# Sparse attention and a rational MLP on one core: fewer, wider transposes, residue-ordered strided V, local X through DRAM, paced casts

## The chip, the cores and the metric

The kernel runs on one core of a Trainium2 chip. The metric is the device time of one execution in microseconds. Five engines work side by side and wait for each other through semaphores: TensorE (PE; its weight loads are listed apart as PEld), VectorE (DVE), ScalarE (ACT), GpSimd (POOL) and SyncE (SP). SP and POOL issue the DMAs; 16 DMA engines carry them out.

## The reference

Attention first, then an MLP on its result. q, k and v have the shape (8 batches, 8 heads, 576 positions, 64).

```python
scores = q @ k.transpose(0, 1, 3, 2) / sqrt(64)
rel = pos[:, None] - pos[None, :]
mask_local   = (rel >= 0) & (rel < 32)                        # heads 0 to 3
mask_strided = (rel >= 0) & (pos[None] % 32 == pos[:, None] % 32)  # heads 4 to 7
attn = softmax(where(mask, scores, -1e9))
x = (attn @ v).transpose(0, 2, 1, 3).reshape(4608, 512)
h = x @ w_in                                                  # 512 -> 2048
P = a0 + a1*h + a2*h**2 + a3*h**3
Q = 1 + |b0|*|h| + |b1|*h**2
out = (P / (Q + 1e-6)) @ w_out                                # 2048 -> 512
```

## The kernel before

All arithmetic on TensorE is in bf16. The inputs are float32 in DRAM, so `casts(b)` has POOL issue casting DMAs from DRAM to DRAM: for the local heads two heads side by side in rows of 128 (`lq`, `lk`: two DMAs each per batch), and in bulk for v and for the strided q and k. `loads(b)` then has SP load a batch into SBUF: four transposes for local q and k (`lqT`, `lkT`), six loads of V windows for the local heads (`vL`, L433), eight transposes for strided q and k (`sqT`, `skT`, one per head; two neighbouring positions lie in one row, so that even and odd positions land in the two halves of the partitions), and 32 small DMAs for strided V (`vS`, L455). Each of those takes, for all four heads, the 18 positions of one residue modulo 32 and puts them on every third partition. POOL then copies strided q into blocks of three residues (`sqP`, L445).

`attention(b)` works through six units: four local heads and two pairs of strided heads. A unit is: a mask matmul and the score matmuls into PSUM (`ps_s`), the row maximum on DVE, its subtraction as a matmul, the exponential on ACT into `pL` or `pS`, a DMA transpose of the probabilities issued by SP (`ptL` L509, `ptS` L564), the product with V into `ps_acc`, and on DVE a reciprocal and a multiplication into `xL` or `xS`. V carries a column of ones, so the product also gives the row sum. Strided X goes from `xS` to DRAM in six POOL stores (`xs`, L592).

`gather(b, xl)` fills `xt`, which holds X transposed for a chunk of 512 tokens: local X by transposes from SBUF in pieces of up to 96 rows (L615, 57 in all), strided X by two transposes per batch from DRAM (L623). There are nine chunks. `mlp1` multiplies a chunk with `Win` in 16 blocks of 128 columns, four matmuls each (L641), ACT copies each block out (L645), and per group of eight blocks nine DVE instructions (L656 to L670) and two on ACT (a logarithm and an exponential in place of the division) work out the rational function. `mlp2` multiplies with `Wout` (L683), ACT copies (L688) and POOL stores the output (L694).

The order on each engine is not the order of the program. Each operation is recorded with an estimated duration, a key and, for a DMA, an estimated transfer time (`P.op`). `schedule` is a planner: it takes for each engine, in estimated time, the ready operation with the smallest key, and so writes down a fixed order per engine. For casts the key is `b * 576 - 1500`, for loads `b * 576 - 700` and a little more, for attention `b * 576` and 96 more per unit, for the MLP of chunk c `c * 512 + 1150` and more. In the planner all DMAs share one queue (`dmafree`), and SP's issues are put at 0.15 us each. Every engine then works its list strictly in order and waits where an operand is late.

Operations depend on each other by tiles. A ring is a number of buffers used in turn; a new use of one waits for the readers of the old. `ps_s` has two buffers, `ps_acc` one, `ptL` and `ptS` two each.

Of the kernel before, what the change touches and what calls it, by code (L numbers as in the profile page):

```python
# [60 lines left out]
class Prog:  # L61
# [34 lines left out]
    def schedule(self):  # L96
# [9 lines left out]
        dmafree = 0.0  # L106
# [131 lines left out]
def bass_strided_sparse_attn__then__act_rational_pade_kernel(nc, q, k, v, moe_w_in, moe_w_out, moe_a, moe_b, out):  # L238
# [57 lines left out]
    R_lqT = ring("lqT", 4, [128, S])  # L296
    R_lkT = ring("lkT", 4, [128, S])
    SW = S // 2 + 16
    R_sqT = ring("sqT", 2, [128, HL, SW])
    R_skT = ring("skT", 2, [128, HL, SW])  # L300
    R_sqP = ring("sqP", 2, [128, HL, NBK, SB])
    R_vL = ring("vL", 2, [128, NTL, HL, 66])
    R_vS = ring("vS", 2, [128, 3, 2, HL, 2, 65])
# [74 lines left out]
    for t in R_sqT.tiles + R_skT.tiles:  # L378
        fill(t, t.t[:, :, S // 2:SW], 0.0, -9e5)


    def casts(b):
        key = b * 576 - 1500 if b else -1e5
        T_lqk[b].new()
        T_sqk[b].new()
        T_v[b].new()

        def local(pair):
            for s_t, d_t in ((q, lq), (k, lk)):
                P.op("pool", lambda e, s_t=s_t, d_t=d_t: e.dma_start(  # L390
                    d_t[b, pair, :, :].rearrange("s (hh d) -> s hh d", hh=2),
                    s_t[b, 2 * pair:2 * pair + 2, :, :].rearrange("hh s d -> s hh d")),
                    4.0, key, w=[T_lqk[b]], dma=2.4)

        def bulk(s_t, d_t, h0, t):
            n = (H - h0) * S * D
            c = 1024
            P.op("pool", lambda e: e.dma_start(
                bass.AP(tensor=d_t, offset=b * n, ap=[[c, n // c], [1, c]]),
                bass.AP(tensor=s_t.tensor, offset=s_t.offset + (b * H + h0) * S * D, ap=[[c, n // c], [1, c]])),  # L400
                1.2, key, w=[t], dma=0.9 * (H - h0) / 4)
        local(0)
        local(1)
        bulk(v, vs, 0, T_v[b])
        bulk(q, sq, HL, T_sqk[b])
        bulk(k, sk, HL, T_sqk[b])

    def weights():
# [5 lines left out]
        for j in range(4):  # L414
            P.op("pool", lambda e, j=j: e.dma_start(
                Wout[:, 4 * j:4 * j + 4, :],
                w_out[512 * j:512 * j + 512, :].rearrange("(a p) n -> p a n", p=128)),
                2.0, -4e4, w=[T_wout], dma=3.3)


    def loads(b):
        key = b * 576 - 700
        st = {}
        for pair in range(2):
            for nm, R, d_t in (("q", R_lqT, lq), ("k", R_lkT, lk)):
                t = R.next()
                st[nm, pair] = t
                P.op("sp", lambda e, t=t, d_t=d_t, pair=pair: e.dma_start_transpose(t.t[:, 0:S], d_t[b, pair, :, :]),  # L428
                     0.15, key + pair, r=[T_lqk[b]], w=[t], dma=0.85)
        vl = R_vL.next()  # L430
        for i in range(NTL):
            w0 = max(0, TQ * i - STRIDE)
            P.op("sp", lambda e, i=i, w0=w0: e.dma_start(  # L433
                vl.t[:, i, :, 0:64], vs[b, 0:HL, w0:w0 + 128, :].rearrange("h p d -> p h d")),
                0.15, key + 5, r=[T_v[b]], w=[vl], dma=0.7)
        st["vl"] = vl
        tq, tk = R_sqT.next(), R_skT.next()
        for h in range(HL):
            for t, d_t in ((tq, sq), (tk, sk)):
                P.op("sp", lambda e, t=t, d_t=d_t, h=h: e.dma_start_transpose(  # L440
                    t.t[:, h, 0:S // 2], d_t[b, h, :, :].rearrange("(c two) d -> c (two d)", two=2)),
                    0.15, key + 10, r=[T_sqk[b]], w=[t], dma=0.43)
        qp = R_sqP.next()
        for h in range(HL):
            P.op("pool", lambda e, h=h: e.tensor_copy(  # L445
                qp.t[:, h, :, :].rearrange("p b (t i) -> p b t i", i=3),
                bass.AP(tensor=tq.t, offset=h * SW, ap=[[HL * SW, 128], [3, NBK], [16, TT], [1, 3]])),
                0.7, key + 11, r=[tq], w=[qp])
        st["sq"], st["sk"] = qp, tk
        vS = R_vS.next()  # L450
        for i in range(16):
            blk, i3 = divmod(i, 3)
            base = 64 * (blk % 2) + i3
            for par in range(2):
                P.op("sp", lambda e, i=i, par=par, blk=blk, base=base: e.dma_start(  # L455
                    vS.t[base:base + 52:3, blk // 2, par, :, blk % 2, 0:64],
                    bass.AP(tensor=vs, offset=((b * H + HL) * S + 2 * i + par) * D,
                            ap=[[32 * D, TT], [S * D, HL], [1, D]])),
                    0.15, key + 12, r=[T_v[b]], w=[vS], dma=0.1)
# [3 lines left out]
    def attention(b, st):  # L463
# [4 lines left out]
        for kind, idx in (("L", 0), ("S", 0), ("L", 1), ("S", 2), ("L", 2), ("L", 3)):  # L468
# [5 lines left out]
            if kind == "L":  # L474
                h = idx
                pb_ = 64 * (h % 2)
                tq, tk = st["q", h // 2], st["k", h // 2]

                def score(e, tq=tq, tk=tk, pb_=pb_, pst=pst):
# [4 lines left out]
                    for i in range(NTL):  # L484
# [11 lines left out]
                def negm(e, ng=ng, pst=pst):  # L496
                    r = None
                    for j, n in ((0, 4), (1, 2)):
# [11 lines left out]
                     0.15, key, r=[pp], w=[pt], dma=0.83)  # L510
# [18 lines left out]
            tq, tk = st["sq"], st["sk"]  # L529

            def score(e, tq=tq, tk=tk, idx=idx, pst=pst):
# [4 lines left out]
                for j in range(2):  # L536
                    for blk in range(NBK):
                        for par in range(2):
                            kc = tk.t[64 * par:64 * par + 64, idx + j, 3 * blk:3 * blk + 288]
# [11 lines left out]
            def negm(e, ng=ng, pst=pst):  # L551
                r = None
                for j in range(2):
# [11 lines left out]
                 0.15, key, r=[pp], w=[pt], dma=1.1)  # L565
            for j in range(2):
# [37 lines left out]
    def gather(b, xl):  # L604
        key = b * 576 + 550
        for i in range(NTL):
            r0 = 0
            while r0 < TQ:
                g0 = b * S + i * TQ + r0
                c, col = divmod(g0, CH)  # L610
                n = min(TQ - r0, CH - col)
                if r0 == 32:
                    n = min(n, 32)
                t = chunk_tile(c)
# [142 lines left out]
```

How the kernel before makes its waits and increments, by code:

```python
            def go(eng):  # L200
                for ws, o in queues[e]:
                    for s, n in ws:
                        eng.wait_ge(s, n)
                    inst = o.maker(eng)
                    if o.dma is not None:
                        inst.then_inc(o.dst.sem, 16)
                    elif inst is not None:
                        inst.then_inc(sems[e], 1)
# [6 lines left out]
        def pool(eng):  # L215
            run("pool")(eng)
            for s, n in fin.items():
                eng.wait_ge(s, n)
```

## Time and profile before

| | |
|---|---|
| Median of three executions | 778.69 us (777.74 to 779.48) |
| Profiled execution | 781.19 us, span 779.0 us, 6110 instructions |
| Busy: PE, DVE, ACT, POOL | 395.9, 362.0, 267.7, 141.1 us |
| Mean granted TensorE clock | 0.861 |
| DMA issues of vS, of xt from xL, of vL | 256, 57, 48 |

Times on the page are microseconds from the first instruction of the profiled execution. Busy time is the time in which an engine had an instruction under way; issuing a DMA from SP is not counted as busy, and stands as SPq. The chain of waits is followed back from the last instruction: at each step to what released it. In a timeline, the name behind an arrow in brackets is what ended the idle time before an instruction. The granted clock is a share of 2.4 GHz, 0.5 being the lower level of 1.2 GHz.

### The profile page before, as it was taken

The numbers are of one execution on the slowest core, as the hardware profiler recorded it, in microseconds if no ns is written. First come the engines' busy times: TensorE is split into PE (matmuls) and PEld (weight loads), VectorE is DVE, ScalarE is ACT, GpSimd is POOL, SyncE is SP. The second block draws the span as 40 slices with busy tenths as digits, with TensorE's granted clock in tenths as the row PEclk, the third lists the DMA queues.
The fourth block names the chain that finished last, engine by engine and source line by source line (L and its number), as shares of the span: only waits on it lengthen the run. The fifth ranks groups of instructions, "written<-read, shape, count | busy, mean of one in ns | idle before, by whom it ended". The sixth has DMA issues, their size and how long they took to land.

```text
span 779.0 us, 6110 instructions
## 1 busy us (share of the span) xinstructions
PE 395.9 (51%) x2304; PEld 178.2 (23%) x2304; DVE 362.0 (46%) x353; ACT 267.7 (34%) x265; POOL 141.1 (18%) x184
## 2 busy tenths in 40 slices
PE   0212240401565010890169095789089959699864
PEld 0001120200222000340024042344034424233321
DVE  3000130100309104360298086489088959969960
ACT  0100000100126040262057044458138657577740
POOL 9007034005160100120003002022010400301100
PEclk9999999999997555795579588799579979999988
DMA  9999969218899042232301342352141321301011
GB/s 148 197 146 116 153 91 111 46 28 127 109 138 123 12 79 53 66 74 39 70 9 53 57 91 48 71 101 60 29 88 30 76 67 39 83 13 55 27 41 40
DMA packets 186076, 58.44 MB, mean 75 GB/s; under 512 B 179552, under 2 KB 182144, under 8 KB 185536
## 3 DMA queue, kind: packets, MB, share of 16 engines
q0 software_dynamic: 46144, 30.17, 23.3%
q1 hardware_dynamic: 139904, 27.90, 22.4%
q8 instruction: 18, 0.29, 0.2%
q14 instruction: 10, 0.08, 0.0%
HBM read 42.54 MB, written 25.95 MB: 88 GB/s over the span
## 4 chain that ended last, share of the span: by engine, by line
SPq 49%; PE 18%; DVE 17%; DMA 6%; ACT 4%; issue 4%; POOL 0%; DVEq 0%; ACTq 0%; POOLq 0%
SPq L455 24%; SPq L440 9%; PE ps_out L683 8%; PE ps_h L641 7%; SPq L615 7%; SPq L433 4%; SPq L428 4%; DVE z L666 3%; DVE z L668 3%; DMA ptL<-pL 3%; DVE h L670 2%; DVE u L660 2%; SPq L509 2%; DVE z L667 1%; ACT u L661 1%
## 5 line engine op out<-in xcount | busy, mean ns | idle before, releaser
L683 PE MATMUL ps_out<-Wout,h 128*128 128x512 bf16 x576 | 148.3, 411 | 25.6 <-ACT os L688 13.1
L641 PE MATMUL ps_h<-xt,Win 128*128 128x512 bf16 x576 | 144.2, 403 | 22.2 <-ACT h L645 9.4
L645 ACT ACTIVATE h<-ps_h 128x512 bf16<-128x512 f32 x144 | 85.0, 597 | 107.4 <-PE ps_h L641 107.3
L516 PE MATMUL ps_acc<-vL,ptL 128*96 128x65 bf16 x192 | 17.5, 237 | 165.3 <-DMA ptL<-pL 163.0
L505 ACT ACTIVATE pL<-ps_s 96x768 bf16<-96x768 f32 x32 | 25.7, 803 | 218.5 <-DMA ptL<-pL 121.4
L522 DVE RECIPROCAL rc<-ps_acc 96x6 f32<-96x6 f32 x32 | 6.1, 189 | 189.0 <-PE ps_acc L516 188.9
L694 POOL DMA_DIRECT2D out_dram<-os x36 | 26.5, 736 | 344.6 <-ACT os L688 340.2
L683 PEld LDWEIGHTS ps_out<-Wout,h 128*128 128x128 bf16 x576 | 57.0, 104 | 103.2 <-issue 17.1
L641 PEld LDWEIGHTS ps_h<-xt,Win 128*128 128x128 bf16 x576 | 52.0, 103 | 98.4 <-ACT h L645 30.4
L661 ACT ACTIVATE u<-u,consts 128x4096 bf16<-128x4096 bf16 x18 | 66.6, 3702 | 2.3 <-DVE u L660 2.2
L663 ACT ACTIVATE u<-u 128x4096 bf16<-128x4096 bf16 x18 | 65.1, 3618 | 0.1
L592 POOL DMA_DIRECT2D xs<-xS x48 | 35.4, 742 | 155.8 <-DVE xS L583 155.7
L493 DVE TENSOR_REDUCE ng<-ps_s 96x6 bf16<-96x768 f32 x32 | 30.3, 946 | 60.7 <-PE ps_s L487 60.6
L516 PEld LDWEIGHTS ps_acc<-vL,ptL 128*96 128x96 bf16 x192 | 15.6, 155 | 174.1 <-DMA ptL<-pL 166.9
L688 ACT ACTIVATE os<-ps_out 128x512 f32<-128x512 f32 x36 | 21.5, 596 | 98.6 <-PE ps_out L683 98.5
L481 PE MATMUL ps_s<-ML,IDN 128*96 128x512 bf16 x64 | 21.2, 423 | 57.4 <-DMA lkT<-lk 31.8
L445 POOL COPY sqP<-sqT 128x324 bf16<-128x324 bf16 x32 | 18.5, 620 | 128.0 <-DMA sqT<-sq 128.0
L390 POOL DMA_DIRECT2D lk<-in_k_dram x16 | 41.4, 3070 | 0.0
L524 DVE TENSOR_TENSOR xL<-ps_acc,rc 96x384 bf16<-96x384 f32 x32 | 17.6, 549 | 51.2 <-DMA xt<-xs 48.7
L660 DVE TENSOR_TENSOR u<-u,z 128x4096 bf16<-128x4096 bf16 x18 | 41.1, 2286 | 0.3
L666 DVE TENSOR_TENSOR z<-z,h 128x4096 bf16<-128x4096 bf16 x18 | 41.0, 2279 | 0.2
L670 DVE TENSOR_TENSOR h<-z,u 128x4096 bf16<-128x4096 bf16 x18 | 41.1, 2282 | 0.1
(41 smaller groups left out, 474.5 us busy)
## 6 DMA issues: line engine op xcount, KB each, us to landing
out_dram<-os POOLq DMA_DIRECT2D x36, 256.0 KB, 2.5
v<-in_v_dram POOLq DMA_DIRECT2D x8, 576.0 KB, 10.3
vS<-v SPq DMA_DIRECT2D x256, 9.0 KB
vL<-v SPq DMA_DIRECT2D x48, 64.0 KB, 2.2
lq<-in_q_dram POOLq DMA_DIRECT2D x16, 144.0 KB, 11.5
lk<-in_k_dram POOLq DMA_DIRECT2D x16, 144.0 KB, 11.3
sq<-in_q_dram POOLq DMA_DIRECT2D x8, 288.0 KB, 10.6
sk<-in_k_dram POOLq DMA_DIRECT2D x8, 288.0 KB, 11.8
```

What stands on the lines that cost most here:

```text
L390: P.op("pool", lambda e, s_t=s_t, d_t=d_t: e.dma_start(d_t[b, pair, :, :].rearrange("s (hh d) -> s hh d", hh=2), s_t[b, 2 * pair:2 * pair ...
L440: P.op("sp", lambda e, t=t, d_t=d_t, h=h: e.dma_start_transpose(t.t[:, h, 0:S // 2], d_t[b, h, :, :].rearrange("(c two) d -> c (two d)", t ...
L455: P.op("sp", lambda e, i=i, par=par, blk=blk, base=base: e.dma_start(vS.t[base:base + 52:3, blk // 2, par, :, blk % 2, 0:64], bass.AP(tens ...
L615: P.op("sp", lambda e, t=t, r0=r0, n=n, col=col, i=i: e.dma_start_transpose(t.t[:, 0:2, col:col + n], xl.t[r0:r0 + n, i, :]), 0.15, key + ...
L641: r = e.matmul(ph.t[:, :], Win[:, kk, f * 128:(f + 1) * 128], xt.t[:, kk, :], start=(kk == 0), stop=(kk == NK1 - 1))
L645: P.op("act", lambda e, f=f, ph=ph, h=h: e.activation(h.t[:, f % G, :], ph.t[:, :], AF.Copy), 0.53, key, r=[ph], w=[h])
L660: dv(lambda e, zz=zz, uu=uu: e.tensor_tensor(uu, uu, zz, op=Alu.mult), tt, r=[z], m=[u])
L661: P.op("act", lambda e, uu=uu: e.activation(uu, uu, AF.Ln, bias=eps1, scale=1.0), 0.833 * W / 1000 + 0.28, key, r=[T_co], m=[u])
L663: P.op("act", lambda e, uu=uu: e.activation(uu, uu, AF.Exp, scale=-1.0), 0.833 * W / 1000 + 0.19, key, m=[u])
L666: dv(lambda e, zz=zz, hh=hh: e.tensor_tensor(zz, zz, hh, op=Alu.mult), tt, r=[h], m=[z])
L670: dv(lambda e, zz=zz, hh=hh, uu=uu: e.tensor_tensor(hh, zz, uu, op=Alu.mult), tt, r=[z, u], m=[h])
L683: r = e.matmul(po.t[:, :], groups[g].t[:, j, m * 128:(m + 1) * 128], Wout[:, kk, :], start=(kk == 0), stop=(kk == NF - 1))
```

## The change

Local q and k of a batch stand in one DRAM tensor (`lqk16`) and come in by one transpose of 2304 rows into `lT`; strided q and k likewise, through `sqk16` into `sT`. V of the local heads is cast in bulk. V of the strided heads is cast by 13 DMAs into `vp16`, whose rows are already in the order of blocks and residues, and six DMAs load it into `vS`. Local X is stored to DRAM by one POOL DMA into the left half of each row of `xs16`, and `gather` has two transposes per batch for whole rows. The casts of batch b + 2 are recorded after attention(b) and wait for the first score of batch b. The rings of `ptL` and `ptS` have three buffers. The planner has one DMA queue per issuing engine, and new durations for SP; the key of the `Wout` loads goes from -4e4 to -300.

```diff
-        dmafree = 0.0
+        dmafree = {e: 0.0 for e in self.ENG}
...
-                dmafree = max(dmafree, t + o.dur) + o.dma
-                o.fin = dmafree + 2.2
+                dmafree[e] = max(dmafree[e], t + o.dur) + o.dma
+                o.fin = dmafree[e] + 2.2
...
-    R_ptL = ring("ptL", 2, [128, NTL, TQ])
-    R_ptS = ring("ptS", 2, [128, 2 * 3, 128])
+    R_ptL = ring("ptL", 3, [128, NTL, TQ])
+    R_ptS = ring("ptS", 3, [128, 2 * 3, 128])
...
+        pace = [first_score[b - 2]] if b - 2 in first_score else []
+
+        def po(fn, dur, t, dma):
+            o = P.op("pool", fn, dur, key, w=[t], dma=dma)
+            for d in pace:
+                o.deps[d] = 1
...
-        bulk(v, vs, 0, T_v[b])
-        bulk(q, sq, HL, T_sqk[b])
-        bulk(k, sk, HL, T_sqk[b])
+        bulk(v, vl16, b * n, 0, n, T_v[b])
+        bulk(q, sqk, b * 2 * n, HL, n, T_sqk[b])
+        bulk(k, sqk, (b * 2 + 1) * n, HL, n, T_sqk[b])
+        vo = b * NBK * SB * HL * 128
+        for h in range(HL):
+            for i3 in range(3):
+                so = v.offset + (b * H + HL + h) * S * D + i3 * 2 * D
+                po(lambda e, h=h, so=so, i3=i3: e.dma_start(
+                    bass.AP(tensor=vp16, offset=vo + (i3 * HL + h) * 128,
+                            ap=[[3 * HL * 128, TT], [SB * HL * 128, 5], [1, 128]]),
+                    bass.AP(tensor=v.tensor, offset=so, ap=[[32 * D, TT], [6 * D, 5], [1, 128]])),
+                    0.75, T_vp[b], 0.25)
+        po(lambda e: e.dma_start(
...
-        for pair in range(2):
-            for nm, R, d_t in (("q", R_lqT, lq), ("k", R_lkT, lk)):
...
-                P.op("sp", lambda e, t=t, d_t=d_t, pair=pair: e.dma_start_transpose(t.t[:, 0:S], d_t[b, pair, :, :]),
-                     0.15, key + pair, r=[T_lqk[b]], w=[t], dma=0.85)
+        lt = R_lT.next()
+        P.op("sp", lambda e: e.dma_start_transpose(
+            lt.t[:, :, :, :].rearrange("p a b s -> p (a b s)"), lqk[b, :, :, :, :].rearrange("a b s d -> (a b s) d")),
+            1.4, key, r=[T_lqk[b]], w=[lt], dma=3.4)
...
-        for h in range(HL):
-            for t, d_t in ((tq, sq), (tk, sk)):
-                P.op("sp", lambda e, t=t, d_t=d_t, h=h: e.dma_start_transpose(
+        P.op("sp", lambda e: e.dma_start_transpose(
+            sT.t[:, 0:2 * HL * SW], bass.AP(tensor=sqk, offset=b * 2 * HL * S * D, ap=[[128, 2 * HL * SW], [1, 128]])),
+            1.4, key + 10, r=[T_sqk[b]], w=[sT], dma=3.4)
...
-        for i in range(16):
-            blk, i3 = divmod(i, 3)
-            base = 64 * (blk % 2) + i3
-            for par in range(2):
+        for blk in range(NBK):
+            base = 64 * (blk % 2)
+            n = SB if blk < 5 else TT
+            hi = base + SB if blk < 5 else base + 52
+            P.op("sp", lambda e, blk=blk, base=base, n=n, hi=hi: e.dma_start(
+                vS.t[base:hi:(1 if n == SB else 3), blk // 2, :, :, blk % 2, 0:64],
+                vp16[b, blk, 0:n, :].rearrange("p (h two d) -> p h two d", h=HL, two=2)),
+                0.7, key + 12, r=[T_vp[b]], w=[vS], dma=0.4)
...
+        P.op("pool", lambda e: e.dma_start(
+            bass.AP(tensor=xs, offset=b * S * Fin, ap=[[Fin, TQ], [TQ * Fin, NTL], [1, 256]]), xl.t[0:TQ, :, :]),
+            1.5, base + 500, r=[xl], w=[T_xs[b]], dma=1.5)
...
-                P.op("sp", lambda e, t=t, r0=r0, n=n, col=col, i=i: e.dma_start_transpose(
-                    t.t[:, 0:2, col:col + n], xl.t[r0:r0 + n, i, :]), 0.15, key + i, r=[xl], w=[t], dma=0.3)
...
-                t.t[:, 2:4, col:col + n], xs[b, r0:r0 + n, :]), 0.15, key + 10, r=[T_xs[b]], w=[t], dma=1.5 * n / 512)
+                t.t[:, :, col:col + n], xs[b, r0:r0 + n, :]), 1.3, key + 10, r=[T_xs[b]], w=[t], dma=3.0 * n / 512)
...
     weights()
-    for b in range(1, B):
-        casts(b)
+    casts(1)
...
+        if b + 2 < B:
+            casts(b + 2)
```

## Rows read from the trace of the kernel before

**Rows 1.** The page: busy time with share and instructions; the chain's shares.
```profile
PE 395.9 (51%) x2304; PEld 178.2 (23%) x2304; DVE 362.0 (46%) x353; ACT 267.7 (34%) x265; POOL 141.1 (18%) x184
...
SPq 49%; PE 18%; DVE 17%; DMA 6%; ACT 4%; issue 4%; POOL 0%; DVEq 0%; ACTq 0%; POOLq 0%
SPq L455 24%; SPq L440 9%; PE ps_out L683 8%; PE ps_h L641 7%; SPq L615 7%; SPq L433 4%; SPq L428 4%; DVE z L666 3%; DVE z L668 3%; DMA ptL<-pL 3%; DVE h L670 2%; DVE u L660 2%; SPq L509 2%; DVE z L667 1%; ACT u L661 1%
```

**Rows 2.** SP's timeline, 143 to 300 us: start, duration of the group, line, operation, count.
```profile
143.79 25.06 SPq L455 DMA_DIRECT2D vS<-v  x32
...
180.46 3.33 SPq L433 DMA_DIRECT2D vL<-v  x6
...
218.88 2.59 SPq L623 DMA_TRANSPOSE xt<-xs  x2
...
290.85 8.91 SPq L615 DMA_TRANSPOSE xt<-xL  x7
```

**Rows 3.** Views by tile, lqT and sqT: issue in ns, least/median/most; first and last start.
```profile
L428 SPq DMA_TRANSPOSE lqT<-lq x16: 1146/1263/11241, 11.2 to 527.9; - x16
...
L440 SPq DMA_TRANSPOSE sqT<-sq x32: 1149/1245/5744, 47.4 to 335.0; - x32
```

**Rows 4.** SP's timeline at the start, 28 to 86 us.
```profile
28.94 12.61 SPq L433 DMA_DIRECT2D vL<-v  x6
...
80.11 5.92 SPq L509 DMA_TRANSPOSE ptL<-pL  x2
```

**Rows 5.** TensorE's timeline: first and third mask matmul, first product, first MLP, late MLP.
```profile
31.80 0.87 PE L481 MATMUL ps_s<-ML,IDN 128*96 128x512 bf16 x2 [31.80 <-DMA lkT<-lk]
...
42.06 0.88 PE L481 MATMUL ps_s<-ML,IDN 128*96 128x512 bf16 x2 [0.90 <-ACT pL L505]
...
89.94 0.69 PE L516 MATMUL ps_acc<-vL,ptL 128*96 128x65 bf16 x6 [20.52 <-DMA ptL<-pL]
...
224.43 15.48 PE L641 MATMUL ps_h<-xt,Win 128*128 128x512 bf16 x64
...
514.68 3.62 PE L683 MATMUL ps_out<-Wout,h 128*128 128x512 bf16 x16
```

**Rows 6.** Windows: length, busy time of PE, PEld, DVE, ACT, POOL; clock, DMA share, GB/s.
```profile
0.00:230.00 230.00, 58.08 (x397) 28.18 (x398) 34.24 (x63) 15.83 (x21) 75.53 (x96) 1.00 0.85 117
230.00:300.00 70.00, 18.13 (x102) 7.50 (x100) 22.84 (x17) 22.93 (x19) 4.77 (x4) 0.63 0.62 71
460.00:700.00 240.00, 180.37 (x1067) 81.75 (x1066) 177.87 (x165) 137.08 (x136) 36.09 (x45) 0.87 0.27 59
690.00:752.00 62.00, 50.49 (x223) 20.26 (x220) 60.91 (x36) 46.42 (x41) 5.98 (x8) 0.97 0.09 34
752.00:779.00 27.00, 14.20 (x56) 5.42 (x56) 0.73 (x1) 2.39 (x4) 2.16 (x4) 0.84 0.10 39
```

**Rows 7.** POOL's timeline: copies of strided q, starts of three casts, stores of strided X.
```profile
60.07 1.78 POOL L445 COPY sqP<-sqT 128x324 bf16<-128x324 bf16 x4 [39.58 <-DMA sqT<-sq]
...
64.12 3.06 POOL L390 DMA_DIRECT2D lk<-in_k_dram  x1
64.91 2.79 POOL L398 DMA_DIRECT2D v<-in_v_dram  x1
65.40 2.79 POOL L398 DMA_DIRECT2D sq<-in_q_dram  x1
...
334.32 3.93 POOL L592 DMA_DIRECT2D xs<-xS  x6 [5.31 <-DVE xS L583]
```

**Rows 8.** DMA view: all packets; issues of strided transposes, count and median us to landing.
```profile
DMA packets 186076, 58.44 MB, mean 75 GB/s; under 512 B 179552, under 2 KB 182144, under 8 KB 185536
...
sqT<-sq SPq DMA_TRANSPOSE x32, 2.5
```

**Rows 9.** Groups of instructions by line: shapes, count, busy us, mean ns, idle time before.
```profile
L683 PE MATMUL ps_out<-Wout,h 128*128 128x512 bf16 x576 | 148.3, 411 | 25.6 <-ACT os L688 13.1
L641 PE MATMUL ps_h<-xt,Win 128*128 128x512 bf16 x576 | 144.2, 403 | 22.2 <-ACT h L645 9.4
```

More of the change, by code:

```diff
@@ L280, in bass_strided_sparse_attn__then__act_rational_pade_kernel @@
     T_v = [Tile(f"v{b}") for b in range(B)]
+    T_vp = [Tile(f"vp{b}") for b in range(B)]
     T_xs = [Tile(f"xs{b}") for b in range(B)]
@@ L295, in bass_strided_sparse_attn__then__act_rational_pade_kernel @@
     T_b = Tile("babs")
[L296 to L300, printed above, removed]
+    R_lT = ring("lT", 2, [128, 2, 2, S])
+    SW = S // 2
+    R_sT = ring("sT", 2, [128, 2 * HL * SW + 16])
     R_sqP = ring("sqP", 2, [128, HL, NBK, SB])
     R_vL = ring("vL", 2, [128, NTL, HL, 66])
-    R_vS = ring("vS", 2, [128, 3, 2, HL, 2, 65])
+    R_vS = ring("vS", 2, [128, 3, HL, 2, 2, 65])
     R_pL = ring("pL", 3, [128, NTL * 128])
     R_pS = ring("pS", 2, [128, 2 * NBK * 64])
-    R_ptL = ring("ptL", 2, [128, NTL, TQ])
-    R_ptS = ring("ptS", 2, [128, 2 * 3, 128])
+    R_ptL = ring("ptL", 3, [128, NTL, TQ])
+    R_ptS = ring("ptS", 3, [128, 2 * 3, 128])
     R_xL = ring("xL", 2, [128, NTL, HL * D])
@@ L377, in bass_strided_sparse_attn__then__act_rational_pade_kernel @@
         fill(t, t.t[:, :], 0.0, -9e5)
-    for t in R_sqT.tiles + R_skT.tiles:
-        fill(t, t.t[:, :, S // 2:SW], 0.0, -9e5)
+    for t in R_sT.tiles:
+        fill(t, t.t[:, 2 * HL * SW:], 0.0, -9e5)
+    first_score = {}
     def casts(b):
@@ L386, in casts @@
         T_v[b].new()
[L388 to L401, printed above, removed]
@@ L402, in casts, with bulk @@
-        local(0)
-        local(1)
-        bulk(v, vs, 0, T_v[b])
-        bulk(q, sq, HL, T_sqk[b])
-        bulk(k, sk, HL, T_sqk[b])
+        T_vp[b].new()
+        pace = [first_score[b - 2]] if b - 2 in first_score else []
[3 more added lines that the diff above has]
+                o.deps[d] = 1
+        def bulk(s_t, d_t, off, h0, n, t):
+            c = n // 128
+            po(lambda e: e.dma_start(
+                bass.AP(tensor=d_t, offset=off, ap=[[c, 128], [1, c]]),
+                bass.AP(tensor=s_t.tensor, offset=s_t.offset + (b * H + h0) * S * D, ap=[[c, 128], [1, c]])),
+                1.0, t, 1.9)
@@ new lines, in casts @@
+        n = HL * S * D
+        for pair in range(2):
+            for qk, s_t in ((0, q), (1, k)):
+                po(lambda e, s_t=s_t, qk=qk, pair=pair: e.dma_start(
+                    lqk[b, qk, pair, :, :].rearrange("s (hh d) -> s hh d", hh=2),
+                    s_t[b, 2 * pair:2 * pair + 2, :, :].rearrange("hh s d -> s hh d")), 3.1, T_lqk[b], 2.4)
+        bulk(v, vl16, b * n, 0, n, T_v[b])
+        bulk(q, sqk, b * 2 * n, HL, n, T_sqk[b])
+        bulk(k, sqk, (b * 2 + 1) * n, HL, n, T_sqk[b])
@@ L476, in attention, with score @@
                 pb_ = 64 * (h % 2)
-                tq, tk = st["q", h // 2], st["k", h // 2]
-                def score(e, tq=tq, tk=tk, pb_=pb_, pst=pst):
+                lt = st["lt"]
+                pr = h // 2
+                def score(e, lt=lt, pr=pr, pb_=pb_, pst=pst):
                     for j, n in ((0, 4), (1, 2)):
@@ L528, in attention @@
                 continue
-            tq, tk = st["sq"], st["sk"]
+            tq, tk = st["sq"], st["sT"]
             def score(e, tq=tq, tk=tk, idx=idx, pst=pst):
@@ L602, in chunk_tile, with gather @@
         return xt_of[c]
-    def gather(b, xl):
+    def gather(b):
         key = b * 576 + 550
[L606 to L614, printed above, removed]
-                P.op("sp", lambda e, t=t, r0=r0, n=n, col=col, i=i: e.dma_start_transpose(
-                    t.t[:, 0:2, col:col + n], xl.t[r0:r0 + n, i, :]), 0.15, key + i, r=[xl], w=[t], dma=0.3)
-                r0 += n
         r0 = 0
@@ L707, in bass_strided_sparse_attn__then__act_rational_pade_kernel @@
             st = loads(b + 1)
-        xl = attention(b, cur)
-        gather(b, xl)
+        attention(b, cur)
+        gather(b)
+        if b + 2 < B:
+            casts(b + 2)
         while nxt < NCH and (nxt + 1) * CH <= (b + 1) * S:
```

60 lines of the change are left out of this document (29 added, 31 removed).

## The prediction

> **What bounds the kernel now.** I read the chain of waits first. Its summary [rows 1] gives 49% of the span to SPq, the time that SP's sequencer needs to issue DMAs; matmuls and VectorE have 18% and 17%. The largest single line is L455, the strided-V pieces, with 24%. So no engine's arithmetic is the bound over the whole run: VectorE is busy for 46% and TensorE for 51% [rows 1].
>
> The timeline of SP [rows 2] says what an issue costs, and the views by tile [rows 3] give its spread. A transpose takes 1.24 to 1.29 us (8.91 / 7 = 1.27 for `xt<-xL`, 2.59 / 2 for `xt<-xs`), a piece of vL 3.33 / 6 = 0.56, a piece of vS 25.06 / 32 = 0.78. The medians are the same for 288 rows (sqT, 1245 ns) and 576 rows (lqT, 1263 ns). One batch therefore occupies SP for: lqT and lkT 4 x 1.27 = 5.1; vL 3.3; sqT and skT 8 x 1.25 = 10.0; vS 25.1; six probability transposes 7.5; 57 / 8 = 7.1 transposes of local X 9.1; two of strided X 2.6. The sum is 62.7 us, eight batches 502 us of the span of 779.0.
>
> Two places show what that does. At the start [rows 4, 5] the first score runs at 31.80, but SP is then busy with vL (12.61 us), with the strided transposes and with vS, so the first probability transpose is issued at 80.11, the first probabilities meet V at 89.94, and the first matmul of the MLP comes at 224.43. In the windows [rows 6] VectorE works 34.24 of the first 230 us, 178 of 240 in the middle (74%), and 60.91 of 62 (98%) in the stretch of MLP alone near the end. That last stretch holds two chunks of the MLP, 31 us each; behind it 27 us are left in which VectorE is done.
>
> **The change, part by part.**
>
> SP. Twelve transposes of q and k become two: 15.1 us becomes 2 x c. The shape, four times the largest here, is not in the trace. Below, c is an issue's 1.25; above, it grows with the rows and is 4 x 1.27 = 5.1. Since a doubling from 288 to 576 rows adds 0.02 us [rows 3], I take 1.4. The 32 vS pieces become 6: each between vL's 0.56 and 54 / 18 of 0.78 = 2.3 us; they move as many runs as a vL piece, so I take 0.7, together 4.2. The 7.1 transposes of xL go, and the two that stay are twice as wide, 1.3 each (at most 2.6). vL (3.3) and the six probability transposes (7.5) stay. The new sum is 2.8 + 4.2 + 3.3 + 7.5 + 2.6 = 20.4 us per batch, 163 us in all, against 502 before. SP stops being the bound. With all upper ends it is 10.2 + 13.8 + 3.3 + 7.5 + 5.2 = 40 us, still under what VectorE needs per batch (below).
>
> POOL. Starts of successive casts lie 0.79 us apart for the local ones (64.12 to 64.91) and 0.49 for the bulk ones; a store of strided X costs 3.93 / 6 = 0.66 [rows 7]. Added per batch are 13 casts of strided V in 72 or 90 short rows, each between 0.49 and 0.79 (I take 0.6: 7.8 us), and one store of local X (0.7). That is 8.5 us per batch on an engine busy for 18% [rows 1]; the cover is its idle time. What stands queued behind: a cast paced by the first score of two batches earlier holds up the sqP copies and stores behind it. Before, casts stood behind the copies the same way, POOL waiting 39.58 us once [rows 7]; bound 0 to 40 us once at the start, 0 taken, because score(0) is early.
>
> DMA. The bytes stay but for local X, 2.4 MB more written, on 58.44 MB [rows 8]. Pacing moves casts of batches 2 to 7 out of the first 230 us, when the engines had a share of 0.85, to where the share was 0.27 [rows 6]. The probability transposes there get slower neighbours; I put that into the utilisation below.
>
> Planner. SP's real durations now stand in its costs, so each queue's order should fit better; DMA is split into two independent queues, which fits worse. I cannot price either from a row: between 0 and the difference of 74% and 98%.
>
> **The start.** The four local casts still come first, so the first score stays at 31.8 (a transpose that lands as a whole could make it 5 us later; weights behind more casts, 5 earlier). vL ends at 41.6 as before, the strided transpose adds 2, and the first probability transpose goes at about 45 instead of 80.1. First use at 45 + 9.8 (80.11 to 89.94) = 55. Strided: sqP was copied at 60.07 [rows 7], behind eight transposes; behind one it comes about eight issues less one earlier, at 60 - 8.8 = 51, and at 56 if the wide one lands late, which I take. Scores follow each other at half of 42.06 - 31.80 [rows 5], two take 10.3; then again 9.8: X is whole at 76. Seven stores (4.6) and a landing (2.5, as sqT's [rows 8]) make 83, two transposes and a landing 88: there the first MLP matmul stands, not at 224. Eight blocks of four matmuls at up to twice 0.226 us [rows 5] later, and a little for the copies, VectorE starts on the MLP at about 105, or 97 if the level is high; I take 97, as its first group is fed while attention of batch 1 keeps TensorE busy. Ends: 75 if DMA clears sooner, 140 if stores wait on POOL.
>
> **What is late next.** VectorE has 362.0 us of work [rows 1]. At 97 it has done the fills and about two batches of attention; the 34.24 us before 230 contained about three, so I subtract 27 and leave 335. TensorE is as loaded: MLP matmuls at the high level take 3.62 / 16 = 0.226 us [rows 5], times 1152 = 260 us; attention has 395.9 - 148.3 - 144.2 = 103 us [rows 1, 9], six eighths of it 78: together 338. Two engines of equal load that feed each other, with transposes between, won't reach the 98% of the MLP stretch; with SP gone they should beat the 74%. I take the middle, 86%: 335 / 0.86 = 390. Sum: 97 + 390 + 27 = 514 us of span. The profiled execution was 781.19 us (2.2 more than its span) and the median is 778.69, so 514 + 2.2 - 2.5 = **514 us** as a median. Ends of the likeliest case: with the early start and 93%, 75 + 335 / 0.93 + 27 = 462 (98% was seen only without attention beside it); 97 + 335 / 0.74 + 27 = 577 above.
>
> The page "DMA: Bandwidth & Descriptors" of the Trainium skill (section "Issuing engines are not separate DMA queues") says that DMAs from several engines interleave on the same 16 DMA engines, and that the issue time saved is usually small beside the transfer. By its second half SP's relief would buy little; the SP rows here speak against that, since 502 us of issue lie mostly on the chain. Its first half speaks against the planner's split queues and for the first rival.
>
> **The rivals.**
>
> 1. The DMA engines become the bound. 60.8 MB must move. With shares scaled to one, the start carried 117 / 0.85 = 138 GB/s and the stretch from 230 to 300 carried 71 / 0.62 = 115 [rows 6]. Then 60.8 MB takes 440 to 529 us, and one chunk (31) and the tail (27) follow the last X, some output stores lying beside: about 500 to 587, 565 at the poor mix. For it: casts now run beside everything. Against it: a share of 0.27 in the middle. Chance 0.18.
>
> 2. TensorE stays at the low level. Between 230 and 300 the granted clock was 0.63 with TensorE busy 18 of 70 us; it was 0.97 in 690 to 752 with 50 of 62 [rows 6]. From 1.2 GHz a matmul takes about twice its 0.226. At a mean granted clock of 0.75, 338 / 0.75 = 451 us; at 90% use 501, plus 97 + 27 = 625; with the VectorE bound still partly beside it, 580 to 640. Against it: fewer long waits. Chance 0.10.
>
> The page "TensorE: Matmul & The Clock Gate" of the Trainium skill (section "Part 1: The HAM clock gate") says that the throttled clock is the default and that activity releases it; by that rule, a denser kernel loses this rival, and the two windows agree with it.
>
> 3. SP stays the bound, because the wide transposes are issued as slowly as their rows: 40 us per batch, and at the start, vL's pieces took 12.61 / 6 = 2.1 us under the cast flood [rows 4]; with that all along, 10 more, 50 per batch. 8 x 50 + 97 + 31 + 27 = 555. Against: medians flat in the rows [rows 3], and 5.1 per four transposes already counts it. Chance 0.06.
>
> 4. Slower: the pacing turns the prefetch into a chain. If POOL holds the casts of batch b+2 behind stores that wait for the end of batch b or b+1, each batch runs cast, landing, transpose, score, attention one behind the other. From cast to first score it took 31.8 us at the start [rows 5], and attention with its issues took at most the 62.7 us of SP: 94.5 per batch, 8 x 94.5 + 31 + 27 = 814. It decides from (778.7 - 58) / 8 = 90 us per batch. For it: POOL issues in order, with 22 more issues between. Against: casts have two batches' lead and 47 us per batch of cover. Chance 0.03.
>
> **How the numbers follow.** The forecast (462 to 577) has 0.62, rival 1 (500 to 590) 0.18, rival 2 (580 to 640) 0.10, rival 3 (about 555) 0.06, rival 4 0.03, and 0.01 for no change. The range runs from 462, where about 0.08 lies below, to 595, where most of rival 2 and all of rival 4 lie above (0.12). About 0.2% is what can be told from no change here: faster 0.96, same 0.01, slower 0.03.
>
> **What would show it.** Right: SPq drops from 49% of the chain to under 15%, with vS in 6 issues of 0.6 to 0.9 us per batch; both wide transposes at 1.3 to 1.6 us; the first MLP matmul between 75 and 110; VectorE at 80 to 92% from there to the tail; DMA share about 0.6 to 0.8, spread evenly. Wrong: first MLP matmul after 140; VectorE waiting on xt or on probability transposes for over 80 us; POOL idle on a pace wait while SP waits for casts; a granted clock under 0.8 from 100 us on; wide transposes of 5 us.

## The result and the profile after

The changed kernel takes 574.52 us in the median of its runs (567.13 to 586.55), against 778.22 before; the ratio is 0.7325, with a 95% interval of 0.7258 to 0.7391. The profiled execution took 567.13 us, with a span of 565.2. Two of its four executions (576.16 and 586.55 us) were slow ones and the ratio is formed without them, so it lies a little under 574.52 / 778.22. The forecast of 514 was 60 us too low, and the range 462 to 595 holds the time.

The page of the changed kernel, to set beside [rows 1]: busy times, then the chain by engine and by line.

```profile
PE 377.1 (67%) x2268; PEld 175.1 (31%) x2304; DVE 363.6 (64%) x351; ACT 265.5 (47%) x265; POOL 235.2 (42%) x296
...
PE 31%; DVE 20%; SPq 16%; ACT 14%; DMA 14%; issue 3%; POOL 1%; POOLq 0%
PE ps_h L648 13%; PE ps_out L690 10%; ACT u L670 5%; SPq L448 5%; ACT u L668 5%; SPq L453 5%; DMA ptS<-pS 4%; DMA ptL<-pL 4%; DMA lT<-lqk 3%; DVE u L667 3%; SPq L468 3%; DVE z L673 2%; ACT h L652 2%; DVE z L675 2%; DVE h L677 2%
```

SPq fell from 49% to 16% of a chain that is 214 us shorter. Its place is taken by TensorE, VectorE and, new at this size, DMA with 14%.

SP's timeline shows the issues of a quiet batch, from 340 us on, and four of the crowded start (as [rows 2, 4]).

```profile
30.68 14.04 SPq L453 DMA_TRANSPOSE sT<-sqk  x1
...
54.36 3.99 SPq L524 DMA_TRANSPOSE ptL<-pL  x3
...
149.01 2.07 SPq L441 DMA_TRANSPOSE lT<-lqk  x1
...
169.78 5.51 SPq L630 DMA_TRANSPOSE xt<-xs  x2
...
340.02 2.43 SPq L453 DMA_TRANSPOSE sT<-sqk  x1
...
343.97 2.04 SPq L441 DMA_TRANSPOSE lT<-lqk  x1
...
358.33 4.70 SPq L468 DMA_DIRECT2D vS<-vp  x6
...
366.49 3.35 SPq L448 DMA_DIRECT2D vL<-vl  x6
...
376.00 3.65 SPq L630 DMA_TRANSPOSE xt<-xs  x2
```

In a quiet batch SP needs 2.4 + 2.0 + 4.7 + 3.4 + 3.7, and six probability transposes at their median of some 1.25, so 23.7 us, where 20.4 was forecast. The views by tile (as [rows 3]: least, median, most, in ns) have the spread: a wide transpose costs 2.0 us at its cheapest and 14 in the crowd, a vS piece 0.74 whether it has 18 or 54 partitions.

```profile
L441 SPq DMA_TRANSPOSE lT<-lqk x8: 2038/4382/13748, 11.0 to 344.0; - x8
...
L453 SPq DMA_TRANSPOSE sT<-sqk x8: 2088/2774/14045, 30.7 to 340.0; - x8
...
L468 SPq DMA_DIRECT2D vS<-vp x48: 739/740/3234, 44.8 to 362.3; - x48
```

The windows (as [rows 6]) cut the run where the forecast cut it: until the first MLP matmul, until VectorE's first MLP instruction, until its last, and the tail.

```profile
0.00:180.00 180.00, 63.87 (x451) 33.40 (x453) 42.33 (x78) 16.83 (x21) 106.67 (x159) 1.00 1.29 147
180.00:197.00 17.00, 12.32 (x41) 4.69 (x39) 0.76 (x3) 5.36 (x9) 6.01 (x11) 0.80 0.98 149
197.00:540.00 343.00, 287.54 (x1725) 131.76 (x1759) 320.49 (x271) 240.92 (x231) 120.32 (x126) 0.96 0.49 90
540.00:565.20 25.20, 13.39 (x54) 5.20 (x53) 0.00 (x0) 2.39 (x4) 2.16 (x4) 0.84 0.11 42
```

After 197 us VectorE is busy for 320.49 of 343 us, 93%, at a granted clock of 0.96: this part is better than forecast. Before it, VectorE has 43 us of work in 197, while the DMA engines have a share of 1.29 until 180 us (the times of packets overlap, since the share passes 1). The start was forecast at 97 us. TensorE's timeline of the start (as [rows 5]) has the steps of that forecast, and POOL's timeline the stores of X.

```profile
21.07 0.88 PE L494 MATMUL ps_s<-ML,IDN 128*96 128x512 bf16 x2 [21.07 <-DMA lT<-lqk]
...
57.02 0.69 PE L531 MATMUL ps_acc<-vL,ptL 128*96 128x65 bf16 x6 [22.07 <-DMA ptL<-pL]
72.54 0.84 PE L494 MATMUL ps_s<-ML,IDN 128*96 128x512 bf16 x2 [14.84 <-DMA lT<-lqk]
...
75.90 0.85 PE L549 MATMUL ps_s<-MS,IDN 128*128 128x384 bf16 x2
...
179.78 3.19 PE L648 MATMUL ps_h<-xt,Win 128*128 128x512 bf16 x7 [1.01 <-DMA xt<-xs]
```

```profile
123.73 1.78 POOL L458 COPY sqP<-sT 128x324 bf16<-128x324 bf16 x4 [16.65 <-DMA sT<-sqk]
125.44 0.79 POOL L604 DMA_DIRECT2D xs<-xL  x1
126.21 3.68 POOL L611 DMA_DIRECT2D xs<-xS  x6
```

The first score came at 21 us (forecast 31.8) and the first product at 57 (55). Then it parts: the strided scores of batch 0 stand in TensorE's order behind a score of batch 1, whose lT lands at 72.5. The stores of X stand on POOL behind the copies for batch 2, which wait 16.65 us for its sT, and the transposes into xt are issued at 169.78, on SP behind the loads of batch 3. The first MLP matmul is at 179.78, not 88. Some 40 us of that lie between the last store of X(0), issued by 130, and its transposes at 169.78: in that time SP works off its list, the loads of batch 3 from 149.01 on among it.

### The profile page after: what moved, and what is told of

The parts are those of the page before. It is cut to its first block, busy times and chain, and to the rows that moved or that the text cites. A ratio compares the mean times of both kernels' runs of the same rounds, so it can differ in the third digit from the quotient of the medians.

```text
span 565.2 us, 5814 instructions
## 1 busy us (share of the span) xinstructions
PE 377.1 (67%) x2268; PEld 175.1 (31%) x2304; DVE 363.6 (64%) x351; ACT 265.5 (47%) x265; POOL 235.2 (42%) x296
## 4 chain that ended last, share of the span: by engine, by line
PE 31%; DVE 20%; SPq 16%; ACT 14%; DMA 14%; issue 3%; POOL 1%; POOLq 0%
PE ps_h L648 13%; PE ps_out L690 10%; ACT u L670 5%; SPq L448 5%; ACT u L668 5%; SPq L453 5%; DMA ptS<-pS 4%; DMA ptL<-pL 4%; DMA lT<-lqk 3%; DVE u L667 3%; SPq L468 3%; DVE z L673 2%; ACT h L652 2%; DVE z L675 2%; DVE h L677 2%
## 5 line engine op out<-in xcount | busy, mean ns | idle before, releaser
L648 PE MATMUL ps_h<-xt,Win 128*128 128x512 bf16 x560 | 141.6, 401 | 26.5 <-ACT h L652 18.7
L690 PE MATMUL ps_out<-Wout,h 128*128 128x512 bf16 x556 | 132.5, 385 | 28.1 <-ACT os L695 13.5
L701 POOL DMA_DIRECT2D out_dram<-os x36 | 34.8, 1177 | 159.0 <-ACT os L695 155.0
L414 POOL DMA_DIRECT2D vp<-in_v_dram x96 | 88.2, 3558 | 0.0
L690 PEld LDWEIGHTS ps_out<-Wout,h 128*128 128x128 bf16 x576 | 54.2, 99 | 94.6 <-ACT os L695 16.9
L458 POOL COPY sqP<-sT 128x324 bf16<-128x324 bf16 x32 | 30.1, 1532 | 89.5 <-DMA sT<-sqk 89.5
L611 POOL DMA_DIRECT2D xs<-xS x48 | 43.8, 1060 | 53.4 <-DVE xS L599 53.4
L675 DVE TENSOR_TENSOR z<-z,h 128x4096 bf16<-128x4096 bf16 x18 | 41.3, 2294 | 0.2
L667 DVE TENSOR_TENSOR u<-u,z 128x4096 bf16<-128x4096 bf16 x18 | 41.1, 2286 | 0.2
L404 POOL DMA_DIRECT2D lqk<-in_k_dram x16 | 41.3, 2923 | 0.0
L673 DVE TENSOR_TENSOR z<-z,h 128x4096 bf16<-128x4096 bf16 x18 | 41.0, 2277 | 0.2
L663 DVE TENSOR_SCALAR z<-h 128x4096 uint16<-128x4096 uint16 x18 | 21.9, 1217 | 24.1 <-ACT h L652 24.1
```

The source lines that it names most:

```text
L404: po(lambda e, s_t=s_t, qk=qk, pair=pair: e.dma_start(lqk[b, qk, pair, :, :].rearrange("s (hh d) -> s hh d", hh=2), s_t[b, 2 * pair:2 * pa ...
L414: po(lambda e, h=h, so=so, i3=i3: e.dma_start(bass.AP(tensor=vp16, offset=vo + (i3 * HL + h) * 128, ap=[[3 * HL * 128, TT], [SB * HL * 128 ...
L611: P.op("pool", lambda e, p0=p0, nb=nb, i3=i3, par=par: e.dma_start(bass.AP(tensor=xs, offset=(b * S + 2 * i3 + par) * Fin + 256, ap=[[32 * ...
L648: r = e.matmul(ph.t[:, :], Win[:, kk, f * 128:(f + 1) * 128], xt.t[:, kk, :], start=(kk == 0), stop=(kk == NK1 - 1))
L667: dv(lambda e, zz=zz, uu=uu: e.tensor_tensor(uu, uu, zz, op=Alu.mult), tt, r=[z], m=[u])
L673: dv(lambda e, zz=zz, hh=hh: e.tensor_tensor(zz, zz, hh, op=Alu.mult), tt, r=[h], m=[z])
```

## The experiments

All ratios are to the kernel before; the changed kernel's is 0.7325 (0.7258 to 0.7391). Two theories for the late start: the planner's order, since its costs for POOL's issues are up to four times the measured ones; or the DMA engines, full with casts and loads of batches that are not needed yet.

**e1_cost.** POOL's costs in the planner as measured.

```diff
-                    ... 3.1, T_lqk[b], 2.4)
+                    ... 0.79, T_lqk[b], 2.4)
...
-                    0.75, T_vp[b], 0.25)
+                    0.62, T_vp[b], 0.25)
...
```

> The changed kernel with POOL's measured issue times in the planner (local cast 0.79 instead of 3.1 us, bulk 0.5 instead of 1.0, strided V 0.62 instead of 0.75, stores 0.79 and 0.63 instead of 1.5 and 0.75). Theory order: VectorE is idle before 180 us because the planner overprices POOL and so puts strided scores, stores of X and xt late; first MLP matmul at about 140 instead of 180, time 530 to 550. Theory flood: the DMA engines are full until 180 us whatever the order; first MLP matmul at 170 or later, time 560 to 580.

Measured: ratio 0.7229 (0.7166 to 0.7291), median 561.35 us. The interval meets that of the changed kernel, so a gain of up to some 2% isn't shown. The first MLP matmul came at 174.28, and VectorE's first MLP instruction at 184.15 instead of 197, with 342 us from there to the end of its last in both. So the costs hold at most 13 of the 100 us by which the start is late.

**e2_two.** No casts for batches 2 to 7.

```diff
     def loads(b):
         key = b * 576 - 700
+        b = b % 2
...
-        if b + 2 < B:
-            casts(b + 2)
```

> The changed kernel with the casts of batches 2 to 7 left out; their loads read the casts of batch 0 or 1, so X is wrong for six batches and all other work is the same. Theory flood: casts fill the DMA engines for the first 180 us; without them the first MLP matmul comes at 110 to 130 and the time is 490 to 520. Theory order: the order is nearly the same, so the first MLP matmul stays at 150 or later and the time at 540 or more.

Measured: 0.6468 (0.6435 to 0.6502), 502.4 us; the first MLP matmul at 120.60. Windows of this run, cut at the same events:

```profile
0.00:120.00 120.00, 48.62 (x368) 25.74 (x368) 31.98 (x58) 13.49 (x17) 47.81 (x77) 1.00 1.10 150
120.00:132.00 12.00, 12.00 (x70) 5.49 (x69) 4.92 (x9) 5.97 (x10) 3.63 (x6) 1.00 0.69 134
132.00:473.00 341.00, 299.97 (x1818) 135.57 (x1817) 323.40 (x285) 243.72 (x234) 79.14 (x90) 0.96 0.39 86
473.00:498.00 25.00, 12.71 (x53) 4.91 (x51) 0.00 (x0) 2.39 (x4) 2.16 (x4) 0.84 0.11 42
```

The middle and the tail are as long as in the changed kernel (341 and 25 us, against 343 and 25); the whole difference of 67 us of span lies before VectorE's first MLP instruction (130.06 against 196.99; the window is cut 2 us behind it). Up to the first MLP matmul the engines moved 120 x 150 = 18.0 MB here and 180 x 147 = 26.5 MB there, at about one rate. So the casts of later batches are what makes the first X late by these 67 us.

How they do it is not settled by this run, for the order did not stay nearly the same, as I had expected it to. SP's timeline of this run:

```profile
111.92 3.35 SPq L631 DMA_TRANSPOSE xt<-xs  x2
115.32 2.66 SPq L442 DMA_TRANSPOSE lT<-lqk  x1
```

Here the transposes of X(0) stand ahead of the lT and the vS of batch 3; in the changed kernel (149.01, then 169.78) they stand behind all its loads, which wait for its casts. Fewer bytes and an earlier place on SP came together; e11_novp, below, comes nearest to parting them.

**e3_nopace.** The wait for the first score is left out.

```diff
-        pace = [first_score[b - 2]] if b - 2 in first_score else []
+        pace = []
```

> The changed kernel without the wait of casts(b) for the first score of batch b-2. If the pacing spreads the casts: the casts go out earlier, DMA share over 1 in the first 150 us, first MLP matmul later than 190, time 580 to 610. If POOL's order alone paces them already (copies of strided q stand between two batches of casts): same within 1%, 560 to 580.

Measured: 0.7381 (0.7353 to 0.7409), no difference shown. That wait paces nothing: in POOL's timeline of this run, as in the changed kernel's, the copies, which wait for sT, already stand between two batches of casts.

**e8_pacex.** Measured costs, and a later pace: the casts of batch b+2 wait for the last multiplication of attention(b).

```diff
-        pace = [first_score[b - 2]] if b - 2 in first_score else []
+        pace = [last_x[b - 2]] if b - 2 in last_x else []
...
```

> The changed kernel with POOL's measured issue times in the planner (as e1_cost) and the casts of batch b+2 waiting for the last multiplication of attention(b) instead of its first score. Theory flood: with only two batches of casts in the way, the first MLP matmul comes at 115 to 135, as in e2_two, and the later casts are hidden: 510 to 530. Rival: the prefetch becomes too short, TensorE waits on lT or vS in every batch after 200 us: 555 or more.

Measured: 0.7648 (0.7603 to 0.7694), slower. The first MLP matmul came at 141.22, but VectorE then worked 87.47 and 81.34 of 120 us in two windows, and POOL waited for the pace, four times and 41.1 us in all. The profiled run, at 603.19 us, is the longest of four and 1.7% over the shortest, which is far less than what lies between 70% and the 93% of the changed kernel.

```profile
180.00:300.00 120.00, 84.44 (x509) 37.72 (x508) 87.47 (x86) 61.88 (x56) 67.54 (x77) 0.84 0.81 118
300.00:420.00 120.00, 84.71 (x532) 39.78 (x530) 81.34 (x80) 58.57 (x58) 55.53 (x71) 0.86 0.84 116
```

```profile
POOL lqk L405 <- DVE xL L540: 41.1, 4, 18.8
```

**e10_pace2.** Measured costs, and the later pace for batches 2 and 3 alone: they wait for the end of attention(0).

```diff
-        pace = [first_score[b - 2]] if b - 2 in first_score else []
+        pace = [last_x[0]] if b in (2, 3) else [first_score[b - 2]] if b > 3 else []
...
```

> As e1_cost, with the casts of batches 2 and 3 alone waiting for the end of attention(0). Theory flood with prefetch kept later: first MLP matmul at 135 to 145 as in e8_pacex, VectorE over 90% busy after 180 as in e1_cost: 525 to 545. Rival: batch 2 then comes late and the time is lost between 180 and 300: 560 or more.

Measured: 0.7514 (0.7458 to 0.757), slower. The first MLP matmul came at 179.98, no earlier than without: casts of two batches then went out together, with a DMA share of 1.42 from 120 to 180. The bytes were moved, not removed: 27.2 MB by the first MLP matmul.

**e11_novp.** No strided V casts for batches 2 to 7.

```diff
+        if b > 1:
+            return
         vo = b * NBK * SB * HL * 128
...
```

> The changed kernel with the 13 casts of strided V left out for batches 2 to 7 (their vS loads read batch 0 or 1, so the strided heads of six batches are wrong). If the new small casts cost by their bytes, a sixth of the casts: 10 to 14 us less, 555 to 565. If short pieces cost much more than their bytes: 30 us less or more, 545 or below.

Measured: 0.7269 (0.721 to 0.7328); not told apart from the changed kernel, with the first MLP matmul at 152.04. The new small casts alone are not what costs the 67 us of e2_two, but they have a part in the start: VectorE's first MLP instruction came at 163 against 197, though X(0)'s transposes still stood behind the lT and the sT of batch 3.

This run also shows that an early first matmul is not yet a short run. From VectorE's first MLP instruction to its last it took 377 us against 342, with the same work. The first loss is chunk 1:

```profile
185.86 3.60 PE L650 MATMUL ps_h<-xt,Win 128*128 128x512 bf16 x8 [14.02 <-DMA xt<-xs]
```

The granted clock over these 377 us was 0.90, against 0.96. Only in e2_two, where casts are gone from the whole run, did the time behind the start stay as short.

**e4_oldvs.** Strided V as before, the rest changed.

```diff
-        for blk in range(NBK):
+        for i in range(16):
+            blk, i3 = divmod(i, 3)
...
+            for par in range(2):
+                P.op("sp", ... 0.78, key + 12, r=[T_v[b]], w=[vS], dma=0.1)
...
```

> The changed kernel with strided V as before: one bulk cast of all V and 32 loads per batch of 0.78 us on SP, with that duration in the planner; the 13 casts per batch on POOL go. SP gets 20 us more per batch (about 41 in all). If SP's occupancy is the bound as long as it nears the 47 us per batch of VectorE: 600 to 650. If SP at 41 us stays hidden and the 13 casts cost as much in the DMA engines: 555 to 585.

Measured: 0.787 (0.783 to 0.7909), 617.27 us. SP's timeline of this run and TensorE's, then waits of PEld: the first row is this run's, the other two are the changed kernel's (us in all, times, longest):

```profile
80.21 26.40 SPq L454 DMA_DIRECT2D vS<-vl  x32
106.66 1.27 SPq L511 DMA_TRANSPOSE ptL<-pL  x1
...
137.16 24.03 SPq L454 DMA_DIRECT2D vS<-vl  x28
161.23 3.33 SPq L617 DMA_TRANSPOSE xt<-xs  x2
```

```profile
109.32 0.69 PE L518 MATMUL ps_acc<-vL,ptL 128*96 128x65 bf16 x6 [28.88 <-DMA ptL<-pL]
...
165.92 3.59 PE L635 MATMUL ps_h<-xt,Win 128*128 128x512 bf16 x8 [25.00 <-DMA xt<-xs]
```

```profile
PEld ps_h L635 <- DMA xt<-xs: 46.9, 5, 25.6
...
PEld ps_acc L531 <- DMA ptL<-pL: 35.7, 6, 22.7
PEld ps_h L648 <- DMA xt<-xs: 7.0, 2, 6.2
```

Two blocks of vS stand on SP ahead of something that TensorE waits for: 26.40 us ahead of a probability transpose, 24.03 ahead of the transposes into xt. The waits for local probabilities did not grow: this run has the one of 28.88 us, the changed kernel 35.7 in all. What grew is the wait for xt, from 7.0 to 46.9 us.

**e5_narrow**, the wide transposes cut into twelve, and **e6_oldx**, local X from SBUF with four buffers for xL.

```diff
-        P.op("sp", lambda e: e.dma_start_transpose(
-            lt.t[:, :, :, :].rearrange("p a b s -> p (a b s)"), ...
+        for pair in range(2):
+            for qk in range(2):
+                P.op("sp", lambda e, ...: e.dma_start_transpose(
+                    lt.t[:, qk, pair, :], lqk[b, qk, pair, :, :]), 1.27, ...
...
```

```diff
-                t.t[:, :, col:col + n], xs[b, r0:r0 + n, :]), 1.3, ...
+                t.t[:, 0:2, col:col + n], xl.t[r0:r0 + n, i, :]), 1.27, ...
...
+                t.t[:, 2:4, col:col + n], xs[b, r0:r0 + n, :]), 1.3, ...
```

> The changed kernel with the two wide transposes per batch cut into twelve as before (4 of 576 rows, 8 of 288), at 1.27 and 1.25 us in the planner. SP gets about 10 us more per batch. If SP has slack now: 560 to 585, as the changed kernel. If SP's occupancy still counts: 600 to 630. The wide transposes took 2.0 to 4.4 us to issue, not 1.4; if that is the DMA queue pushing back, the narrow ones will add up to the same per batch.

> The changed kernel with local X transposed from SBUF in 57 pieces as before (1.27 us each in the planner), and four buffers for xL. SP gets about 9 us more per batch, the DMA engines 2.4 MB less. SP has slack: 560 to 580. SP counts: 590 to 620, with VectorE or PE waiting on xt.

Measured: 0.74 (0.7349 to 0.7451) and 0.7268 (0.7236 to 0.73). Neither is told apart from the changed kernel.

**e9_joint.** Both at once.

> The changed kernel with both e5 and e6: twelve narrow transposes and 57 transposes of local X from SBUF. SP gets about 19 us more per batch, as much as the old strided V gave it in e4_oldvs. If what e4 lost is SP's occupancy as such: 605 to 625, as e4. If it is the block of 32 issues ahead of a probability transpose, 25 us at a stretch: 570 to 585, as e5 and e6 alone.

Measured: 0.7381 (0.7313 to 0.7449), 577.79 us, again not told apart. SP's timeline of this run:

```profile
94.05 2.71 SPq L584 DMA_TRANSPOSE ptS<-pS  x2
...
130.87 11.10 SPq L636 DMA_TRANSPOSE xt<-xL  x8
...
148.82 5.13 SPq L443 DMA_TRANSPOSE lT<-lqk  x4
153.99 10.97 SPq L456 DMA_TRANSPOSE sT<-sqk  x8
```

With vS (4.7), vL (3.1), two xt (2.6) and the probabilities (7.5) that is 45 us per batch, as much as in e4_oldvs, where vS takes 25 and the rest some 19. But it costs nothing that these runs can show, and e4 costs 43 us in the median. So the occupancy of SP as such has stopped to count at this size. What e4 has and e9 has not are the waits for xt (46.9 us against 1.3). That the place of the vS blocks ahead of xt costs the 43 us is read from these waits; no run kept e4's loads and moved them.

**b1_spcost.** The kernel before, with SP's measured issue times in the planner and four buffers for xL; no DMA is changed.

```diff
-                    0.15, key + 12, r=[T_v[b]], w=[vS], dma=0.1)
+                    0.78, key + 12, r=[T_v[b]], w=[vS], dma=0.1)
...
```

> The kernel before with SP's measured issue times in the planner (1.24 to 1.29 us for transposes, 0.55 for vL, 0.78 for vS instead of 0.15), and four buffers for xL; no DMA changed. If the kernel before was bound by SP's occupancy of 502 us: 740 to 780, hardly faster. If a good part was the order that the planner wrote with SP at 0.15 us: 620 to 700.

Measured: 0.9146 (0.9111 to 0.9182), 712.84 us, between the two ranges expected. Its chain still is SP's:

```profile
SPq 46%; PE 24%; DVE 17%; DMA 5%; ACT 4%; issue 3%; POOL 0%; POOLq 0%
SPq L455 22%; PE ps_h L641 13%; PE ps_out L683 7%; SPq L440 7%; SPq L615 6%; SPq L428 5%; SPq L433 4%; DVE z L668 3%; DVE z L666 3%; DVE h L670 3%; DMA xt<-xs 2%; DVE u L660 2%; DVE z L667 2%; DVE z L664 1%; DVE z L656 1%
```

So honest costs and the buffers, which were not tried apart, bring 66 of the 204 us with every DMA as before. What fell is TensorE's wait for local probabilities, while its wait for xt from xs rose, from 8.1 to 58.5 us. The first row is from the kernel before, the second from this run:

```profile
PE ps_acc L516 <- DMA ptL<-pL: 163.0, 10, 23.8
...
PE ps_acc L516 <- DMA ptL<-pL: 42.7, 4, 16.8
```

**e12_cshared.** e1_cost with one DMA queue in the planner, as before the change.

```diff
-        dmafree = {e: 0.0 for e in self.ENG}
+        dmafree = 0.0
...
```

> As e1_cost, with one DMA queue for all engines in the planner again, as before the change. If the 16 DMA engines are shared in fact, the planner's order gets better: 540 to 553. If its one queue is too strict (all transfers one after another, probability transposes behind casts): 570 to 600.

Measured: 0.7387 (0.733 to 0.7444), against 0.7229 (0.7166 to 0.7291) for e1_cost: some 12 us more, with the intervals apart. But VectorE's first MLP instruction is earlier here (178.6 against 184.2); the time is lost behind it, at a granted clock of 0.91 against 0.96, and the two kernels ran on different chips. That one queue per issuing engine writes the better order is not shown.

## Why the prediction was in its range and 60 us too low

**What bounded the kernel before: right in the main.** SP's issues did, but not by their sum alone. With the planner's costs put right and the 62.7 us per batch left in place, the kernel stays at 713 us with 46% SPq; a third of the gain came without taking one issue from SP, and by the waits it came from what its issues stand ahead of. Of the three changes to DMAs, only the undoing of vS costs time that shows (e4_oldvs, 43 us); the wide transposes and local X through DRAM together do not (e9_joint).

**SP's sum: right in its effect, a little low.** 23.7 us per quiet batch, forecast 20.4. The wide transposes cost 2.0 to 2.4 there, not 1.4, inside the bounds of 1.25 and 5.1; in the crowd single ones took up to 14, which no bound had. Rival 3 is out: e9_joint gives SP 45 us per batch and loses nothing that shows.

**The start: the step that failed.** It was put together as a chain of SP issues, at 97 us, with an end at 140 for a wait on POOL. Measured 197, and the first MLP matmul after 140 was my own sign of being wrong. The first product at 57, forecast 55, is luck: the first score came 11 us earlier than forecast, the first probability transpose 9 us later (54.36), and 2.7 us instead of 9.8 passed from there to the product. What I left out is that everything behind them shares the DMA engines, and the lists of POOL and SP, with later batches: the casts of batches 2 and 3 stand on POOL ahead of the stores of X(0), the loads of batches 2 and 3 and the wait for their casts on SP ahead of its transposes; a share of 1.29 until 180 us, 26.5 MB. I took the casts out of the first 230 us by the pacing, and e3_nopace shows that the pacing does nothing. And I put POOL's wait at 0; the copies waited 16.65 us for sT, with the stores of X(0) behind them.

e2_two shows the size: without those casts, VectorE's first MLP instruction is at 130, so 67 of the 100 us are theirs; the other 33 are not explained by a run. In the changed kernel and its variants the rate until the first MLP matmul was 136 to 158 GB/s, and by and large it came later where more bytes went ahead: 18.1 MB at 120.6 us (e2_two), 21.0 at 141.2 (e8_pacex), 23.6 at 152.0 (e11_novp), 26.4 at 179.8 (the changed kernel), but 27.5 at 174.3 (e1_cost). That fits the bytes as the cause. But they go ahead because the orders of POOL and SP put them there, and no run moved X's stores and transposes ahead of them with the casts in place.

**Utilisation: mis-sized the other way.** 93% from 197 to 540, not 86%; the term 335 / 0.86 = 390 measured 343, with 320 us of VectorE's work left. The tail of 27 measured 25. So 197 + 343 + 25 = 565 stands against 97 + 390 + 27 = 514: the start cost 100 us more, the rest 49 less. That the range held is owed to this second error: at the forecast 86% the same start would have given 197 + 320 / 0.86 + 25 = 595, its very end.

**Rival 1 was half true.** Its price, 565, is the span that came, but by luck: its own sum gives 587 at the poor mix, and its mechanism did not hold over the whole run: the DMA engines were full for the first 180 us, and after 197 their share is 0.49 and VectorE's work sets the end. The first half of what the page "DMA: Bandwidth & Descriptors" of the Trainium skill says in "Issuing engines are not separate DMA queues", that DMAs of several engines interleave on the same 16 DMA engines, fits the start (147 and 150 GB/s with 26.5 and 18.0 MB); its second half, that the issue time saved is usually small beside the transfer, does not fit SP's 49% of the chain of the kernel before.

**Rival 2 is out.** The granted clock is 0.96 from 197 to 540, where the kernel before had a mean of 0.861. **Rival 4** did not happen, but e8_pacex shows its beginning: with the casts held back by about one attention more, VectorE falls to about 70% after the start. (POOL got 112 instructions more, 14 per batch, not the 22 counted there.)

**The planner.** I said that split DMA queues fit worse; e12_cshared gives no sign of that, and does not show the contrary. And I priced honest costs between nothing and a share of the utilisation, where b1_spcost, with its buffers, gives 66 us.

**Still open.** How much of the late start is bytes and how much is order, and whether 1.29 of DMA share at the start and 0.49 in the middle can be evened out without losing the prefetch: two paces were tried, both slower. e8_pacex, e11_novp and e12_cshared began the MLP 18 to 45 us earlier than the changed kernel and were not faster. e1_cost is the fastest complete kernel in the median (561.35 us), but its interval meets that of the changed kernel.

## What to carry to other kernels

A queue that only issues DMAs can bound a kernel; what it cost here was less its sum than what its issues stood ahead of: probabilities in the kernel before, X in e4_oldvs. When such a bound goes, ask which bytes and which issues stand ahead of the first result that the next engine needs: the prefetch of several batches was paid there. An earlier first matmul is worth something only if what follows comes earlier too. And a planner's costs are part of the kernel: measure them with it.

## What the hardware showed that was not expected

A DMA issue from SP for 54 partitions took as long as one for 18 (740 ns). A transpose of 2304 rows took 2.0 us to issue where one of 576 took 1.26, so four in one still save 3 us (5.13 for four narrow ones in e9_joint). One such issue, begun at 30.68, held SP for 14 us; from 20 to 40 us the DMA share was 1.52.
